# Attention with a relative-position bias, then a mixture of experts: the bias part's loads in another order, and the second pair's rounding on another engine

## What is computed

```python
scores = scale * np.matmul(q, k.transpose(0, 1, 3, 2))      # B=4, H=8, S=576, D=64
x = (log1p(|i - j|) / log1p(max(i, 1)))[..., None]          # i, j: positions
bias = np.maximum(x @ w1 + b1, 0.0) @ w2                    # hidden 32, then 8 heads
attn = softmax(scores + bias)                               # 1e-9 added to the row sums
x = (attn @ v), heads side by side                          # 2304 tokens x 512
P = eight rounds of row and column scaling of exp(x @ w_gate - max)   # 2304 x 8
out = sum over e of P[:, e] * (relu(x @ w1[e]) @ w2[e])     # 8 experts, 512 -> 1024 -> 512
```

## Time and profile before

| | us |
|---|---|
| median of the runs (lowest, highest) | 1844.34 (1844.29, 1845.65) |
| profiled execution | 1844.29 |
| its span, first to last instruction | 1842.5 |
| TensorE busy in the span | 1826.9 (99%) |
| VectorE busy | 1054.5 (57%) |
| ScalarE busy | 824.6 (45%) |
| GpSimd busy | 1028.1 (56%) |

### The profile page before, as it was taken

The page is one execution under the profiler, slowest core; times in us unless marked ns, Lnnn a source line. Parts: engine busy times, 40 slices in busy tenths (PEclk is TensorE's granted clock), DMA queues, the critical chain, the costliest instruction groups (busy, mean ns, idle before and its releaser), DMA issues.

```text
span 1842.5 us, 27892 instructions
## 1 busy us (share of the span) xinstructions
PE 1826.9 (99%) x10223; PEld 1590.0 (86%) x10223; DVE 1054.5 (57%) x1784; ACT 824.6 (45%) x1416; POOL 1028.1 (56%) x720
## 2 busy tenths in 40 slices
PE   8999999999999999999999999999999999999999
PEld 4677777798999999999999999999999999999998
DVE  8877777778554555456545554555465545544553
ACT  8877777533433333344333333333333333333331
POOL 0223326577666666666776666666666666666661
PEclk9999999999999999999999999999999999999999
DMA  7764562021111111112121122121121111111210
GB/s 229 243 150 97 129 148 68 23 92 53 65 67 69 69 69 69 69 69 103 69 69 69 69 69 69 69 69 69 70 103 69 69 69 69 69 69 69 69 46 35
DMA packets 44127, 152.47 MB, mean 83 GB/s; under 512 B 9584, under 2 KB 18032, under 8 KB 29680
## 3 DMA queue, kind: packets, MB, share of 16 engines
q1 hardware_dynamic: 44016, 150.99, 25.5%
HBM read 135.63 MB, written 15.34 MB: 82 GB/s over the span
## 4 chain that ended last, share of the span: by engine, by line
PE 95%; DVE 1%; ACT 0%; POOL 0%; issue 0%; POOLq 0%; DVEq 0%
PE banks L660 14%; PE banks L661 14%; PE banks L659 14%; PE banks L627 13%; PE banks L631 13%; PE banks L629 13%; PE banks L557 4%; PE banks L518 3%; PE banks L500 3%; PE banks L501 2%; PE banks L571 1%; PE banks L528 0%; PE banks L678 0%; ACT probs L786 0%; DVE x_lo_rest_r L1081 0%
## 5 line engine op out<-in xcount | busy, mean ns | idle before, releaser
L1279 POOL TENSOR_TENSOR w_lo<-stage,w_hi 128x1024 fp32r<-128x1024 f32 (+1 forms) x288 | 647.4, 2264 | 525.7 <-ACT w_hi L832 524.7
L1161 DVE TENSOR_TENSOR u<-p_copy,banks 128x384 f32<-128x384 f32 x192 | 106.3, 554 | 632.0 <-PE banks L631 632.0
L661 PE MATMUL banks<-w_hi,h_lo 128*128 128x512 f32 x1152 | 450.1, 391 | 0.0
L660 PE MATMUL banks<-w_lo,h_hi 128*128 128x512 f32 x1152 | 449.9, 391 | 0.0
L659 PE MATMUL banks<-w_hi,h_hi 128*128 128x512 f32 x1152 | 449.0, 390 | 0.0
L1167 DVE SCALAR_TENSOR_TENSOR h_lo<-corner,h_hi 128x384 fp32r<-128x384 f32 x384 | 412.7, 1102 | 0.0
L879 ACT ACTIVATE h_hi<-corner 128x384 fp32r<-128x384 f32 x384 | 196.5, 526 | 270.9 <-DVE corner L1161 267.9
L627 PE MATMUL banks<-x_hi,w_hi 128*128 128x384 f32 x896 | 300.6, 335 | 0.0
L631 PE MATMUL banks<-x_hi,w_lo 128*128 128x384 f32 x896 | 300.2, 335 | 0.0
L832 ACT ACTIVATE w_hi<-stage 128x1024 fp32r<-128x1024 f32 (+1 forms) x288 | 271.6, 974 | 8.8 <-POOL stage L1273 8.8
L868 ACT ACTIVATE p_copy<-banks 128x384 f32<-128x384 f32 x96 | 47.4, 493 | 491.0 <-PE banks L631 491.0
(11 more groups left out here) (130 smaller groups left out, 2472.2 us busy)
## 6 DMA issues: line engine op xcount, KB each, us to landing
stage<-in_expert_w SPq DMA_DIRECT2D x96, 1024.0 KB, 4.8
raw<-in_qk SPq DMA_DIRECT2D x32, 576.0 KB, 7.2
bias_scratch<-bias_out SPq DMA_DIRECT2D x36, 288.0 KB, 2.6
bias<-bias_scratch SPq DMA_DIRECT2D x16, 288.0 KB, 2.9
v_main<-in_v SPq DMA_DIRECT2D x16, 256.0 KB, 2.7
bias<-bias_scratch SPq DMA_DIRECT2D x16, 256.0 KB, 3.8
out<-total SPq DMA_DIRECT2D x4, 768.0 KB, 4.0
out<-total SPq DMA_DIRECT2D x6, 256.0 KB, 2.0
```

Of the source, the lines that this page charges most:

```text
L660: pe.matmul(dst, h_hi[:, g % 2, f, tokens], lo[:, f], start=False, stop=False)
L661: mm = pe.matmul(dst, h_lo[:, g % 2, f, tokens], hi[:, f], start=False, stop=fp == FPAIRS - 1 and f == 1)
L1161: dve.tensor_tensor(out, other, bank, op).then_inc(combined, 1)
L1279: pool.tensor_tensor(lo, of, hi.bitcast(F32), ALU.subtract).then_inc(w_split, 1)
```

## The change

The diff, cut to its core; what is left out are the declarations of semaphores and the repacked input arrays.

```diff
+SECOND_PAIR_AT = ((1, 5), (5, 7), (7, BIAS_TILES // ROUND - 1))
+TABLE_FIRST = LTAB - S - GROUPS * GROUPS * ROUND
...
-            params = sb("params", [P, 2 + GROUPS * H], F32, inner)
+            params = sb("params", [P, 2 + GROUPS * H + ROW_SETS], F32, inner)
...
 # SyncE
-            for dst, src in [(table[:], log_table), (params[:], bias_w), (slopes[:], inv_psi)]:
-                sp.dma_start(dst, src).then_inc(consts_in, 16)
+            for i, cols in enumerate((slice(TABLE_FIRST, LTAB), slice(0, TABLE_FIRST))):
+                sp.dma_start(table[:, cols], log_table[:, cols]).then_inc(table_in[i], 16)
...
             load_pair(0, 0)
-            load_values(0, 0)
-            load_pair(0, 1)
...
                         for slot in range(ROUND):
                             store_tile(i * ROUND + slot, slot)
+                if qc == 0:
+                    load_pair(0, 1)
+                    load_values(0, 0)
                 for slot in range(ROUND):
                     sp.wait_ge(bias_stored[slot], 16 * min(rounds * (qc + 1), BIAS_TILES // ROUND))
                 load_bias(0, qc)
...
 # TensorE
-            pe.wait_ge(consts_in, 48)
+            pe.wait_ge(params_in, 16)
...
-                if qc == 0:
+                first = not exists(hp, s - 1)
+                if qc == 0 and not first:
                     pe.wait_ge(split_done, 2 * n + 2)
-                if not exists(hp, s - 1):
-                    pe.wait_ge(bias_evac, BIAS_TILES - 2)
+                if not exists(hp, s - 3) and exists(hp, s - 2):
+                    pe.wait_ge(split_done, 2)
                 for h in range(2):
-                    if exists(hp, s - 1):
+                    if first:
+                        if h == 0:
+                            pe.wait_ge(first_split, 2)
+                        else:
+                            pe.wait_ge(split_done, 1)
+                        pe.wait_ge(bias_evac, BIAS_TILES - ROUND + h + 1)
+                    else:
                         pe.wait_ge(biased, 2 * at + h - 1)
...
 # ScalarE
-            act.wait_ge(consts_in, 48)
+            act.dma_start(params[:], bias_w).then_inc(params_in, 16)
+            act.wait_ge(ones_set, 1)
+            act.activation(col_sum[:, 0:1], ones[:, 0:1], ACT.Relu).then_inc(warm, 1)
+            act.wait_ge(params_in, 16)
+            act.wait_ge(table_in[0], 16)
...
             for m in range(ROUND):
+                if m + AHEAD == ROUND:
+                    act.wait_ge(table_in[1], 16)
                 hidden_units(m + AHEAD, (m + AHEAD) % ROUND, again=m + AHEAD >= ROUND)
                 keep_bias(m, m, again=False)
...
-            with act.Fori(1, BIAS_TILES // ROUND - 1) as i:
-                for slot in range(ROUND):
-                    hidden_units(ROUND * i + slot + AHEAD, (slot + AHEAD) % ROUND)
-                    keep_bias(ROUND * i + slot, slot)
+            for begin, end in SECOND_PAIR_AT:
+                with act.Fori(begin, end) as i:
+                    for slot in range(ROUND):
+                        hidden_units(ROUND * i + slot + AHEAD, (slot + AHEAD) % ROUND)
+                        keep_bias(ROUND * i + slot, slot)
+                if end < BIAS_TILES // ROUND - 1:
+                    round_pair(1, 1, SECOND_PAIR_AT.index((begin, end)))
...
 # VectorE
-            dve.wait_ge(consts_in, 48)
             dve.memset(shift[:], 0.0).then_inc(shift_kept, 1)
             dve.memset(row_sum[:], 1.0).then_inc(bias_prep, 1)
-            dve.tensor_scalar(slopes[:], slopes[:], w1_col, None, ALU.mult).then_inc(bias_prep, 1)
+            dve.wait_ge(params_in, 16)
+            dve.tensor_scalar(slopes[:], inv_psi, w1_col, None, ALU.mult).then_inc(bias_prep, 1)
...
+            dve.wait_ge(table_in[0], 16)
             for m in range(ROUND):
                 hidden_units(m, m)
+            dve.wait_ge(table_in[1], 16)
...
-            dve.wait_ge(attn_consts_in, 16)
             dve.wait_ge(rounded, 2)
-            dve.tensor_tensor(qk_hi[0][D:2 * D, 0, :, :], raw[D:2 * D, 0, 0, :, :],
-                              qk_hi[0][D:2 * D, 0, :, :].bitcast(F32), ALU.subtract).then_inc(split_done, 1)
-            dve.tensor_tensor(k_lo[0][:, :, :], raw[:, 0, 1, :, :], qk_hi[0][:, 1, :, :].bitcast(F32),
-                              ALU.subtract).then_inc(split_done, 1)
+            def split_first_queries(cols, done):
+                low = slice(D, 2 * D)
+                dve.tensor_tensor(qk_hi[0][low, 0, :, cols], raw[low, 0, 0, :, cols],
+                                  qk_hi[0][low, 0, :, cols].bitcast(F32), ALU.subtract).then_inc(done, 1)
+            split_first_queries(slice(0, 2 * P), first_split)
+            for h in range(2):
+                dve.tensor_tensor(k_lo[0][:, h, :], raw[:, 0, 1, h, :], qk_hi[0][:, 1, h, :].bitcast(F32),
+                                  ALU.subtract).then_inc(first_split if h == 0 else split_done, 1)
...
 # VectorE, in a step, after both heads' bias
+                if exists(hp, s) and not exists(hp, s - 1):
+                    split_first_queries(slice(2 * P, S), split_done)
...
             for s in range(STEPS):
                 step(0, s)
-                if s < 2:
-                    dve.wait_ge(raw_in[1], 32)
-                    dve.tensor_copy(qk_hi[1][:, :, s, :], raw[:, 1, :, s, :]).then_inc(rounded, 1)
...
 # GpSimd, split_pair
+                pool.wait_ge(split_done, 2 * n)
```

More of the change, by code:

```diff
@@ L80, in main, with bass_attention_moe @@
     return 0 if h == 0 else S + REST
-def bass_attention_moe(nc, qk, v, bias_w, gate_w, expert_w, log_table, inv_psi, identity, out):
+def bass_attention_moe(nc, qk, v, bias_w, gate_w, expert_w, log_table, identity, out):
     with ExitStack() as ctx:
@@ L174, in bass_attention_moe @@
         h_lo = sb("h_lo", [P, 2, 2, 2 * T], F32R)
-        consts_in = sem("consts_in")
+        params_in = sem("params_in")
+        table_in = [sem(f"table_in{i}") for i in range(2)]
+        warm = sem("warm")
         attn_consts_in = sem("attn_consts_in")
@@ L191, in bass_attention_moe @@
         split_done = sem("split_done")
+        first_split = sem("first_split")
         scores_ready = sem("scores_ready")
@@ L336, in bass_attention_moe @@
         w1_col, b1_col, w2_diag = params[:, 0:1], params[:, 1:2], params[:, 2:2 + GROUPS * H]
+        inv_psi = params[:, 2 + GROUPS * H:2 + GROUPS * H + ROW_SETS]
         def halves(ap):
@@ L1372 @@
     arrays = {
-        "qk": qk, "v": vv, "bias_w": bias_w.reshape(P, 2 + GROUPS * H), "gate_w": moe_w_gate,
-        "expert_w": expert_w, "log_table": log_table, "inv_psi": inv_psi, "identity": identity,
+        "qk": qk, "v": vv, "bias_w": np.concatenate([bias_w.reshape(P, 2 + GROUPS * H), inv_psi], axis=1), "gate_w": moe_w_gate,
+        "expert_w": expert_w, "log_table": log_table, "identity": identity,
     }
```

## The result

The changed kernel takes **1848.41 us**, the median of 16 runs (1847.84 to 1848.84), against 1844.32 before (16 runs): +4.1 us, a ratio of 1.0021 with the interval 1.0013 to 1.0028. It is slower. The forecast was 1845.8 with a range up to 1848.5: the sign of the sum and the mechanism hold, the size is 2.6 us too small, and the result lies beyond the 0.2% that the forecast called "the same". I had given that side 0.14.

A forecast was written before the change was run, and what follows sets the result against it. TensorE holds 95% of the chain, so the end moves with attention's start, set by ScalarE and VectorE ahead of 75 us. First scores +1.7 and first steps -0.2 gave +1.5 on 1844.29: 1845.8 us, range 1841.3 to 1848.5.

The forecast's parts named there:

- the same: Whole kernel: no change by the 0.2% (3.7 us) that a measurement can tell; chance 0.82.
- The place and the price of the stall: Eviction of tile 16: store 12 lands at 38.0 behind the moved loads, so ScalarE stands still for 6.1 us.
- the loads cost less: Rival at store 12: it lands before 34 and VectorE's chain decides, 1841.4 us; chance 0.22.
- ScalarE to tile 16: ScalarE's bias part: tile 4 at 15.3, tile 11 at 25.0, tile 16 at 31.9 if nothing held it.
- the start: Start of the kernel: VectorE's units from 4.4, 1.05 earlier; ScalarE from 4.35 instead of 6.69, 2.3 earlier.
- First scores: Start of attention: released by ScalarE at 63.0 instead of 61.30, +1.7 us.
- First steps: Attention's first steps: casts leave VectorE, query low parts and a late fourth reload take some back; net -0.2 us.
- From 75 us on nothing changes: Rest of the kernel after 75 us: the same length, 0 us.
- The sum: +1.7 - 0.2 = +1.5 on the profiled execution's 1844.29: 1845.8 us.
- slower by over 0.2%: Whole kernel above 1848.0 us, from most of the slow rival and part of the warm-up; chance 0.14.
- one mechanism with a landing after 40.2: Slow rival at store 12: reload served late, landing 40.5, scores at 65.5, +4.2, 1848.5 us; chance 0.12.

The follow-up runs named there:

- e2: Kernel before with only the loads of pair 1 and the first values moved behind the first 12 stores; 1848.03 us, ratio 1.0017.
- e1: Changed kernel with the old order of loads, first values and pair 1 right behind pair 0; 1844.40 us, ratio 0.9999.
- e5: Changed kernel with only pair 1 behind the 12th store and the first values behind the 16th; 1847.08 us, ratio 1.0013.
- e3: Changed kernel with the moved loads spread: halves of pair 1 behind the 4th and 8th stores, values behind the 16th; 1842.90 us, ratio 0.9990.
- e9: e3 with the first two loads of expert weights (2 MB) moved behind the first head pair; 1842.65 us, ratio 0.9990.
- e11: e2 with eight idle matmuls, which change no result, put ahead of TensorE's tile 19; 1848.04 us.
- e10: e9 with GpSimd doing the rounding of pair 1 and all low parts of pair 0 during the bias part; 1847.29 us, ratio 1.0014.
- e4: Changed kernel with pair 1 issued on ScalarE's queue instead of SyncE's and the values behind the 16th store; 1845.45 us, ratio 1.0004.

## Why the prediction came out as it did

- **The place and the price of the stall: right.** The forecast put a wait of 6.1 us at tile 16, from the pair's and values' 7.2 us in one queue and the reload's 309 GB/s; it measured 6.17. In the changed kernel the pair's second half, issued at 28.0, landed 8.0 us later, at 36.0, the large piece of the values at 36.1, and their last 16 KB at 37.1; the forecast's 35.1, moved by the 0.9 by which the loads were issued later, is 36.0. e2 shows that it makes 3.7 of the 4.1 us, e1 that without it the change costs nothing, e5 that it follows what stands ahead. The Trainium skill's 341 GB/s, by which the result would have been 2.9 us better, is not what these loads do, and it was the wrong line to hold against them: it is told of loads over 128 partitions, and each of pair 1's two spans 64. For 64 partitions the Trainium skill ("SBUF — State Buffer", Door 1: The DMA port swizzle) gives 196 GB/s for 1 MiB. The trace agrees with that, as 1152 of the 1440 KB are such loads: 1440 KB in 7.2 us are 205 GB/s. The rival "the loads cost less" falls by the landing of store 12, at 39.1 and not before 34.
- **"ScalarE to tile 16", the start: mis-sized by 1.0.** The forecast had ScalarE at 4.35 and tile 4 at 15.3; they came at 4.70 and 16.33. The params landed 3.4 us after their issue and not 3.1 (0.35 in all). I had let ScalarE evict tile 0 as soon as it had its own units done. It waited 0.68 us for TensorE, whose first matmuls ran at half speed. With 0.2 more between tile 4 and tile 16 this is tile 16 at 39.22 instead of 38.0, and tile 32 at 63.45 instead of 62.2.
- **"First scores", the step that failed: +0.5.** I let the scores follow the eviction of tile 32. TensorE has first to finish bias tile 35, whose fourth group needs ScalarE's last hidden unit (62.70, 0.92 us long), so that it ended its bias work at 64.8. The change's earlier wait (tile 32 for the first head), counted in the forecast at 0.7, brings about 0.1: tile 33 was out at 64.86, and TensorE's own order held the scores until 64.76.
- **"First steps": -0.2 forecast, +0.3 measured.** The casts' 1.4 us are gone, but only the one in step 0 stood on the way to step 3, and the 0.85 us of low parts took its place. The cast in step 1 moved step 2 (70.19, +3.1) and not step 3 (72.99, +3.8): from step 1 to step 3 it takes 4.96 us without the cast and 4.97 with it (68.03 and 64.24), since step 3 hangs on the transposes of step 1. The fourth reload, for which I had charged a part, wasn't late.
- **"From 75 us on nothing changes": +0.3.** Pair 2's load lands later, since SyncE's queue is later as a whole. e3 shows such a wait plainly, 0.80 us, and e9 takes it away. In the changed kernel it is 0.2 at most, and the rest of the 0.3 stays open.
- **The sum.** 1.25 + 0.5 + 0.5 + 0.3 is 2.6, what the forecast fell short by. VectorE's stall was put at a quarter of the wait at most, and at nothing in its 58.8; it was 2.7 us. TensorE's clock made much of it, if it acts here as in e2, where e11 takes the waits from 3.45 to 1.30. The stall stayed hidden, since VectorE's low parts for the first head were ready at 62.0.

The forecast gave "slower by over 0.2%" mostly to one mechanism with a landing after 40.2. It came there by four small terms, all on the side of later, with the landing at 39.1. The range holds the result only because it was drawn for that other mechanism. It should have taken the terms beside the stall as uncertain, too: each was taken near its best case.

## What to carry to other kernels

A load that is moved "behind the stores" stands ahead of the next ones: price it by the buffer that the next store frees, and cut it into pieces that fit the slack of one slot. Here the same bytes cost 6.2 us in one block and nothing in three pieces behind different rounds of stores, and the version in pieces (e3) takes 1.4 us less than the kernel before and 5.5 less than the changed one; with the weights later (e9) it is 1.7 and 5.8. When a wait in front of a matmul is relaxed, look first at what that engine itself still has to do before it.

## What the runs showed of the hardware

- **TensorE's clock after idleness.** Mean granted clock 0.53 from 40.0 to 43.4 us, the level of 1.2 GHz, after 4.6 us in which TensorE did nothing; 0.50 in e2 after 5.2, and 1.00 with most of that gap filled (e11). In e10 it is 0.50 from 63.0 to 67.5, after 4.0. Matmuls as slow as these stand at the start of every run (684 to 687 ns), though the clock column reads 1.00 there: at the start the clock is seen in the durations alone, and "1.0 throughout" in the section on the profile before rests on that column. Mean time of the bias matmuls in three stretches of the changed kernel (the groups by line, ns of one behind the comma):

```profile
L473 PE MATMUL banks<-hidden,params 128*32 128x288 f32 x26 | 3.6, 686 | 1.3 <-DVE hidden L1012 1.3
```

```profile
L473 PE MATMUL banks<-hidden,params 128*32 128x288 f32 x48 | 4.7, 412 | 0.0
```

```profile
L473 PE MATMUL banks<-hidden,params 128*32 128x288 f32 x24 | 3.5, 684 | 4.6 <-DVE hidden L1012 4.6
```

  686 ns at first, 412 at full clock, 684 after the stall. How long the slow start lasts differs between profiled runs of the same work: from 9.5 to 11.5 us they took 421 ns in the changed kernel and still 686 in e5, whose ScalarE waited 0.42 and 0.18 us more for TensorE. The wait of 0.68 us at tile 0, which the kernel before did not have, is where part of the early start went.
- **VectorE shuts GpSimd out.** While VectorE ran its back-to-back single-source units, a GpSimd subtraction made no end for 44 us (e10). It ended 2.5 us after VectorE's last unit, and alone it takes 2.66. That is one instruction in one run, and no run varied VectorE's units beside it. The reverse did not show: from 20 to 50 us VectorE's units took 0.578 us beside it and 0.581 in e9 without it. The Trainium skill ("SBUF — State Buffer", Who interferes with whom) has the two engines share a pair of ports that one instruction holds alone, whichever was first, when VectorE runs in a mode that uses both pairs; whether these units run in it, no row shows. The trace agrees with the exclusion, by the 44.03 us; that GpSimd, too, holds VectorE up did not show. An idle engine is not a free one.
- **Queues on two engines share one service time** (e4), and ScalarE's sequencer issues a DMA ahead of the work that stands before it in the program: the issue at 24.25 belongs behind the eviction of tile 11, which started at 26.18. Where a load is to come late, it needs a wait.
